# Attention with a fused mixture of experts: the value products of a batch in two bursts instead of five

## The reference, cut to what matters

```python
# attention: batch 4, heads 8, sequence S = 576, head size 64, all float32
scores = q @ k.T / 8 + bias              # bias depends on (head, query, key)
scores = scores - max(scores, axis=-1)
attn = exp(scores)
attn = attn / (sum(attn, axis=-1) + 1e-9)
x = (attn @ v)                           # then heads side by side: 2304 tokens x 512
# mixture of experts on x: 8 experts, hidden 1024, soft routing
logits = x @ w_gate;  P = exp(logits - max)
for _ in range(8): P /= rows(P) + 1e-9;  P /= columns(P) + 1e-9;  P *= N / E
out = sum_e P[:, e] * (relu(x @ w1[e]) @ w2[e])
```

## Time and profile before

| | us |
|---|---|
| three runs | 1845.45, 1845.69, 1844.3 (median 1845.45) |
| the profiled execution | 1844.29 |
| its span | 1842.5 |
| TensorE busy in the span | 1826.9 |
| VectorE, ScalarE, GpSimd busy | 1054.5, 824.6, 1028.1 |

### The profile page before, as it was taken

How to read it: one execution, slowest core, us unless ns; L and a number is a source line. 1 busy time by engine, 2 the same in 40 slices (tenths; PEclk the granted TensorE clock), 3 DMA queues, 4 the chain that set the end, 5 groups by cost and what they waited for, 6 DMA issues and landing times.

```text
span 1842.5 us, 27892 instructions
## 1 busy us (share of the span) xinstructions
PE 1826.9 (99%) x10223; PEld 1590.0 (86%) x10223; DVE 1054.5 (57%) x1784; ACT 824.6 (45%) x1416; POOL 1028.1 (56%) x720
## 2 busy tenths in 40 slices
PE   8999999999999999999999999999999999999999
PEld 4677777798999999999999999999999999999998
DVE  8877777778554555456545554555465545544553
ACT  8877777533433333344333333333333333333331
POOL 0223326577666666666776666666666666666661
PEclk9999999999999999999999999999999999999999
DMA  7764562021111111112121122121121111111210
GB/s 229 243 150 97 129 148 68 23 92 53 65 67 69 69 69 69 69 69 103 69 69 69 69 69 69 69 69 69 70 103 69 69 69 69 69 69 69 69 46 35
DMA packets 44127, 152.47 MB, mean 83 GB/s; under 512 B 9584, under 2 KB 18032, under 8 KB 29680
## 3 DMA queue, kind: packets, MB, share of 16 engines
q1 hardware_dynamic: 44016, 150.99, 25.5%
HBM read 135.63 MB, written 15.34 MB: 82 GB/s over the span
## 4 chain that ended last, share of the span: by engine, by line
PE 95%; DVE 1%; ACT 0%; POOL 0%; issue 0%; POOLq 0%; DVEq 0%
PE banks L660 14%; PE banks L661 14%; PE banks L659 14%; PE banks L627 13%; PE banks L631 13%; PE banks L629 13%; PE banks L557 4%; PE banks L518 3%; PE banks L500 3%; PE banks L501 2%; PE banks L571 1%; PE banks L528 0%; PE banks L678 0%; ACT probs L786 0%; DVE x_lo_rest_r L1081 0%
## 5 line engine op out<-in xcount | busy, mean ns | idle before, releaser
L1279 POOL TENSOR_TENSOR w_lo<-stage,w_hi 128x1024 fp32r<-128x1024 f32 (+1 forms) x288 | 647.4, 2264 | 525.7 <-ACT w_hi L832 524.7
L1161 DVE TENSOR_TENSOR u<-p_copy,banks 128x384 f32<-128x384 f32 x192 | 106.3, 554 | 632.0 <-PE banks L631 632.0
L661 PE MATMUL banks<-w_hi,h_lo 128*128 128x512 f32 x1152 | 450.1, 391 | 0.0
L660 PE MATMUL banks<-w_lo,h_hi 128*128 128x512 f32 x1152 | 449.9, 391 | 0.0
L659 PE MATMUL banks<-w_hi,h_hi 128*128 128x512 f32 x1152 | 449.0, 390 | 0.0
L1167 DVE SCALAR_TENSOR_TENSOR h_lo<-corner,h_hi 128x384 fp32r<-128x384 f32 x384 | 412.7, 1102 | 0.0
L879 ACT ACTIVATE h_hi<-corner 128x384 fp32r<-128x384 f32 x384 | 196.5, 526 | 270.9 <-DVE corner L1161 267.9
L627 PE MATMUL banks<-x_hi,w_hi 128*128 128x384 f32 x896 | 300.6, 335 | 0.0
L631 PE MATMUL banks<-x_hi,w_lo 128*128 128x384 f32 x896 | 300.2, 335 | 0.0
L832 ACT ACTIVATE w_hi<-stage 128x1024 fp32r<-128x1024 f32 (+1 forms) x288 | 271.6, 974 | 8.8 <-POOL stage L1273 8.8
L868 ACT ACTIVATE p_copy<-banks 128x384 f32<-128x384 f32 x96 | 47.4, 493 | 491.0 <-PE banks L631 491.0
(11 more groups left out here) (130 smaller groups left out, 2472.2 us busy)
## 6 DMA issues: line engine op xcount, KB each, us to landing
stage<-in_expert_w SPq DMA_DIRECT2D x96, 1024.0 KB, 4.8
raw<-in_qk SPq DMA_DIRECT2D x32, 576.0 KB, 7.2
bias_scratch<-bias_out SPq DMA_DIRECT2D x36, 288.0 KB, 2.6
bias<-bias_scratch SPq DMA_DIRECT2D x16, 288.0 KB, 2.9
v_main<-in_v SPq DMA_DIRECT2D x16, 256.0 KB, 2.7
bias<-bias_scratch SPq DMA_DIRECT2D x16, 256.0 KB, 3.8
out<-total SPq DMA_DIRECT2D x4, 768.0 KB, 4.0
out<-total SPq DMA_DIRECT2D x6, 256.0 KB, 2.0
```

The source lines that it names most:

```text
L660: pe.matmul(dst, h_hi[:, g % 2, f, tokens], lo[:, f], start=False, stop=False)
L661: mm = pe.matmul(dst, h_lo[:, g % 2, f, tokens], hi[:, f], start=False, stop=fp == FPAIRS - 1 and f == 1)
L1161: dve.tensor_tensor(out, other, bank, op).then_inc(combined, 1)
L1279: pool.tensor_tensor(lo, of, hi.bitcast(F32), ALU.subtract).then_inc(w_split, 1)
```

## The change

```diff
-PV_PARTS = ((4, 0, range(0, 3), False), (5, 0, range(3, 5), True),
-            (6, 1, range(0, 2), False), (7, 1, range(2, 3), False), (8, 1, range(3, 5), True))
-PV_DONE = (2, 5)
+PV_PARTS = ((4, 0, range(0, 5), False), (6, 1, range(0, 5), False))
+PV_DONE = (1, 2)
+HEADS_AT = (5, 7)
...
                 for half in range(2):
-                    after = PV_PARTS[PV_DONE[half] - 1][0]
-                    if (s - after) % QC == 0 and exists(hp, s - after):
-                        keep_heads(hp, s - after, half)
+                    if (s - HEADS_AT[half]) % QC == 0 and exists(hp, s - HEADS_AT[half]):
+                        keep_heads(hp, s - HEADS_AT[half], half)
```

## The result

The changed kernel takes 1861.8 us, the median of four runs (1860.3 to 1861.9), against 1844.88 of the kernel before in four runs of its own: a ratio of 1.0091, with a 95% interval of [1.0078, 1.0104]. It is slower, by 16.9 us in the medians. The two profiled executions, both at the full clock from end to end, lie 1860.30 - 1844.29 = 16.0 apart.

The account below looks back on a forecast made before the run. TensorE bounds the attention only while its steps cover the other engines' chains. First batch +1.0, fourteen batches +14.1, last batch 0 and tail +1.3 sum to +16.4 us; forecast 1861.5, range 1851 to 1867.

Parts of the forecast that it names:

- TensorE's own work: TensorE's blocks in steps 0 to 4 of a batch, without waits: 16.44 us with the change, against 17.28 before.
- the 0.84 saved: TensorE's saving per attention batch from three bursts fewer, 0.28 us each: 17.28 - 16.44.
- Step 1's wait: Transposes of step 1 wait for ScalarE's copy of the turned 64-row block from uncovered step 0: 0.82 us a batch.
- Step 3's wait: Spreading piece 0 of the inverses waits for VectorE's rest copy: 0.51 us a batch, 0.42 from the heads copy ahead.
- Step 4's waits: Piece 1 waits 0.09 us for VectorE's rest copy, then the transposes 0.43 for ScalarE's copy, its exponentials held by rounding.
- The sum: Per attention batch: 16.44 us of TensorE work plus 1.85 lost in waits gives 18.29, against 17.28: +1.01.
- GpSimd just ahead of becoming the bound: GpSimd's splits let the next batch's scores start at about 18.0 us, just ahead of 18.29: no cost here.
- only step 0's wait is real: Rival: waits behind the rounding are hidden; +0.1 us a batch, +3 in all, about 1848; chance 8%.
- The ends: First batch +1.0 us, last batch 0, tail +1.3 as the wait before piece 1 grows from 1.00 to about 2.3.
- How the page would count it: Chain of waits over the attention: some 18 us for ScalarE's copy, some 7 for VectorE's rest copy.
- The clock rival: Three gaps a batch bring TensorE's clock to 1.2 GHz, doubling 16.4 us of work a batch: up to +260; chance 2%.
- the rival of the other side: TensorE alone bounds the kernel; three bursts' fixed cost, 13.4 us, is saved, giving about 1833; chance 6%.

Follow-up runs that it names:

- run 1: Kernel before, with only half 0's value products gathered in one burst behind step 4's transposes, half 1 in three bursts as before: 1853.2 us, ratio 1.0046.
- run 2: Kernel before, with only half 1 in one burst behind step 6's transposes and its heads copy in step 7: 1863.07 us, ratio 1.01.
- run 3: Changed kernel with the heads copy of half 1 back in step 8, behind the copies it was put ahead of: 1858.83 us.
- run 4: Changed kernel with ScalarE copying the turned block between the exponentials of head 0 and head 1, not behind both: 1851.21 us, ratio 1.0034.
- run 6: run 3 with both of ScalarE's roundings of the next batch in step 1 instead of one each in steps 1 and 2: 1853.8 us, ratio 1.005.
- run 5: Kernel before with a sixth burst: step 1's two chunks issued one ahead of the transposes and one behind them: 1848.99 us, ratio 1.0025.
- run 7: Against the kernel before, three bursts, in steps 0, 1 and 3, with heads copies in steps 5 and 8: 1863.83 us, ratio 1.0107.
- run 8: run 7 with both of ScalarE's roundings in step 1: 1838.79 us, ratio 0.997 against the kernel before.
- run 10: Two bursts, in steps 0 and 2, each ahead of its step's transposes, both roundings in step 1: 1838.86 us, ratio 0.9966 against the kernel before.
- run 11: run 10 with ScalarE copying the turned block between its two exponentials: 1838.05 us, ratio 0.996 against the kernel before.
- run 12: run 11 with VectorE's last two factor splits in the tail moved from behind step 7 to behind step 10: 1835.96 us, ratio 0.9954 against the kernel before.
- run 9: Control: kernel before with its five bursts and both of ScalarE's roundings in step 1: 1844.2 us, ratio 0.9996.

## Why the prediction was right

The forecast was 1861.5, against 1861.8; the sum for the profiled execution was +16.4, against +16.0 measured. The mechanism is the one forecast, and runs 1 to 4 and 6 show it; that the batch came out within 0.01 us is luck: the work was put 0.09 too low and the waits 0.09 too high. Step by step:

- **TensorE's own work, 16.44 a batch.** Near, and 0.1 too low: the blocks of the changed kernel, each without its wait, add up to 16.53 (the blocks that wait taken from the kernel before). The prediction took 1.16 from the scores of step 0 to what follows, and they take 1.25, in the kernel before as well (230.34 to 231.60 in its timeline). It also read the batch of the earlier trace rows as free of waits. There the transposes of step 4 take 246.13 - 244.78 = 1.35 to the burst, which the walk put at 1.12 without a word; the changed kernel takes 1.10. Over fourteen batches the mean before is 1.22, so some 0.1 of the 0.84 saved is a wait that the change covers. The gain of a burst less was put at 0.28; run 5 measured 0.25 to 0.30 for one more, and the blocks give 0.65 for three fewer (17.29 less that 0.1, against 16.53), 0.22 each. The formula of the Trainium skill, TensorE: Matmul & The Clock Gate, section Back-to-back issue gap, which the page gives for an isolated matmul, has no term for it; the trace of run 5 decides against leaving it out.
- **Step 1's wait, 0.82.** It was 0.71 in the mean. The moment at which the transposes could start was right (3.84 behind the batch's first scores, 3.81 measured); TensorE only came to them 0.09 later, for the 1.25 above. The mechanism is shown by runs 1 and 4.
- **Step 3's wait, 0.51.** It was 0.39 in the mean, with 0.39 instead of 0.28 between the spreading and the transposes (0.31 in the kernel before). I had given 0.42 of it to the moved heads copy; run 3 shows that this is true of the wait and not of the time, since ScalarE's copy comes out at the same moment.
- **Step 4's waits, 0.09 and 0.43.** They were 0.05 and 0.46 in the mean. Run 6 shows the rounding as the cause of the second.
- **The sum, 1.85 lost and 18.29 a batch.** 18.29 measured, as 16.53 of work and 1.76 lost.
- **GpSimd just ahead of becoming the bound.** Right, and closer than I used: run 2 crossed the line with half of the change, and run 7 by 1.7 us a batch (18.57 against 16.89 of run 8). The rival "only step 0's wait is real" had left this out of its price; what GpSimd would have cost such a version was not run.
- **The ends.** First batch +1.0: 75.95 - 61.30 = 14.65 against 13.67. The tail's wait 2.3: 2.34. From the last batch's first scores to the end the profiles are 1.1 apart, where the sum had 1.3.
- **How the page would count it.** Wrong in size: I expected 18 us for ScalarE's copy and 7 for VectorE's, and the rows give 13.4 and 4.1. The difference is in the counting, since the page's idle times leave out 0.12 to 0.17 of each wait and all short ones: the starts give 0.71 x 15 + 0.46 x 14 = 17.1 and 0.39 x 15 = 5.9.
- **The clock rival.** In the profiled execution it did not happen, with three waits a batch: 1.00 over the whole attention. In the three other runs of the changed kernel the mean clock was 0.999, and they took 1.5 us more; where it fell in them no trace shows. That single falls, of 1.5 us each, happen behind longer waits was in no rival; they are told below. The clock is 0.9 of the 16.9 us of the medians (1861.8 and 1844.88 each mix runs at the full clock with others).

That TensorE alone was the bound (the rival of the other side) is false for the places this change chose, and true for those of runs 8 and 10 to 12.

## What to carry to other kernels

An engine that is 99% busy is also the cover for everything behind it: before work is gathered, find for each step the chain that must come out by its end, and leave each step as long as that chain. Fewer, longer bursts did gain here once they stood ahead of the instruction that waits, and once the instruction that fed the next chain (ScalarE's rounding for GpSimd) moved to where there was cover. Walking one period with durations and hand-over times from the trace gave each wait and block to about 0.1 us, enough to tell 18.3 from 17.3; that the sum was off by only 0.01 is chance. And a wait that is taken away can leave another of nearly its size right behind it (runs 3, 6 and 11), so a saving is to be read from the start of the burst that follows, not from the wait.

## What the runs showed of the hardware

I had not expected the clock to play a part. Run 11's TensorE timeline at the end of the attention:

```profile
333.57 0.52 PE L571 MATMUL banks<-ident,inv_wide 128*128 128x128 f32 x3 [2.35 <-DVE x L1027]
...
334.10 0.34 PE L629 MATMUL banks<-x_lo_first_r,w_hi 128*128 128x384 f32 x1
334.28 0.49 PE L631 MATMUL banks<-x_hi,w_lo 128*128 128x384 f32 x1
334.57 0.52 PE L627 MATMUL banks<-x_hi,w_hi 128*128 128x384 f32 x1
...
337.75 0.34 PE L629 MATMUL banks<-x_lo_rest_r,w_hi 128*128 128x384 f32 x1
```

Behind an idle time of 2.35 us the matmuls take 0.52 where their like takes 0.33 or 0.34, from 334.3 to 337.7, so the fall comes 0.7 us after the wait is over. Run 10's profile has two such places (columns: stretch, its length, busy time and count of each engine, granted clock, transfers' share, GB/s):

```profile
64.00:68.00 4.00, 4.00 (x24) 3.98 (x24) 3.00 (x8) 3.01 (x8) 0.00 (x0) 0.65 0.78 205
68.00:72.00 4.00, 3.06 (x23) 2.50 (x22) 4.00 (x11) 2.68 (x6) 3.21 (x2) 1.00 1.01 420
...
336.00:340.00 4.00, 3.55 (x13) 3.58 (x14) 1.35 (x3) 0.00 (x0) 0.00 (x0) 0.57 0.00 0
340.00:344.00 4.00, 4.00 (x25) 4.00 (x24) 1.82 (x3) 3.31 (x6) 1.48 (x1) 1.00 0.00 0
```

The clock was at its lower level (1.2 GHz) for most of 64 to 68 us, in the first batch, after idle times of 1.58 and 0.44, and again behind the tail's wait. The length of the idle time does not settle whether it falls. The profiles of runs 4 and 5 have the fall in the first batch too, and those of the changed kernel and of runs 1, 2, 3, 6, 8, 9 and 12 have the 1.58 without it. A tail's wait of 2.34 or 2.35 brought it in the profiles of runs 2, 10 and 11, and not in those of the changed kernel and run 4. Nor does it happen in each execution of one kernel: run 10's six runs took 1837.85 to 1838.33 at a mean clock of 1.000, 1839.39 and 1839.97 at 0.999, and 1840.96 at 0.998. One fall costs about 1.5 us, two cost 3. The kernel before has it in some runs too (1844.2 to 1844.6 and 1845.4 to 1846.1), and none of run 9's ten has it. The waits of 0.2 to 0.7 in each steady batch of the changed kernel brought no fall in its profiled run. The Trainium skill, TensorE: Matmul & The Clock Gate, section A second HAM failure mode: psum-queue depth-cycling, tells of a clock that swings where TensorE idles a little between groups; the steady part here does not bear that out. The falls in the traces stand behind single longer waits. Run 7 waits ahead of the scores of fourteen batches, thirteen times for 1.44 to 1.67 and once for 2.07. It spread furthest, 1860.74 at a mean clock of 1.000 to 1866.88 at 0.996, and in its profile the clock fell once, at the wait of 2.07. Run 12, which cut the tail's wait from 2.35 to 0.67, was at 0.999 in two of five runs, run 11 in four of five. That fits a fall behind the longer waits; it is too few runs to call it shown, and what else must be there for a fall was not settled.
